# VectorE's softmax tail of one tile moved ahead of the next tile's head

## What is computed

```python
scores = scale * np.matmul(q_c, k_c.transpose(0, 1, 2, 4, 3))
scores = scores - np.max(scores, axis=-1, keepdims=True)
attn = np.exp(scores)
attn = attn / (np.sum(attn, axis=-1, keepdims=True) + 1e-09)
out = np.matmul(attn, v_c)
...
x = out.transpose(0, 2, 1, 3).reshape(B * S, H * D)      # 2304 tokens x 512
# experts: P from x @ w_gate, exp, 8 Sinkhorn steps; out += P[:, e] * (relu(x @ w1[e]) @ w2[e])
# last block: elu(x @ w_in) @ w_out, d_ff = 2048
```

## Time and profile before

| | |
|---|---|
| time, median of 3 runs | 1995.28 us (1994.5 to 1996.69) |
| time of the profiled execution | 1994.76 us |
| its span | 1993.0 us |
| busy in the span: PE, DVE, ACT, POOL | 98%, 56%, 36%, 27% |
| first matmul of the first expert step | 82.66 us from the span's start |

### The profile page before, as it was taken

One profiled execution on the slowest core, in us unless ns is written; L12 is line 12 of the kernel. 1 busy time (PEld: TensorE's weight loads), 2 busy tenths in 40 slices (PEclk: granted clock), 3 DMA queues, 4 the chain that ended last, 5 costly groups with the idle time before them and its releaser, 6 DMA issues.

```text
span 1993.0 us, 30945 instructions
## 1 busy us (share of the span) xinstructions
PE 1946.3 (98%) x10450; PEld 1752.8 (88%) x10450; DVE 1118.8 (56%) x1874; ACT 719.7 (36%) x1516; POOL 531.0 (27%) x600
## 2 busy tenths in 40 slices
PE   6799999999999999999999999999999989999999
PEld 5699999998999889998899988999889868998888
DVE  6666654555545555455554555545555576666666
ACT  4632223322232323332223322233323455555554
POOL 4822252222222222222222222222222352222220
PEclk9999999999999999999999999999999999999999
DMA  9310000000000000000000000000000000000002
GB/s 225 84 36 29 22 22 22 21 21 21 21 21 21 21 21 31 27 26 21 21 21 21 21 21 21 21 21 21 21 21 32 11 22 22 21 21 21 21 21 95
DMA packets 34264, 61.37 MB, mean 31 GB/s; under 512 B 3248, under 2 KB 21680, under 8 KB 34224
## 3 DMA queue, kind: packets, MB, share of 16 engines
q1 hardware_dynamic: 34224, 60.84, 10.4%
HBM read 56.12 MB, written 4.72 MB: 31 GB/s over the span
## 4 chain that ended last, share of the span: by engine, by line
PE 93%; DVE 3%; POOL 2%; ACT 1%; issue 1%; POOLq 0%; DVEq 0%
PE bank L480 44%; PE bank L510 8%; PE bank L497 8%; PE bank L498 8%; PE bank L502 8%; PE bank L511 8%; PE bank L512 8%; POOL prob L312 1%; DVE x_sum L972 1%; POOL x_lo L366 1%; ACT x_hi L718 0%; PE bank L583 0%; DVE x_lo L983 0%; DVE acc L1008 0%; DVE acc L1002 0%
## 5 line engine op out<-in xcount | busy, mean ns | idle before, releaser
L480 PE MATMUL bank<-x_hi,w_hi 128*128 128x384 f32 x1680 | 568.0, 338 | 10.9 <-DVE x_lo L983 6.9
L480 PE MATMUL bank<-x_hi,w_lo 128*128 128x384 f32 x1680 | 565.8, 337 | 0.0
L480 PE MATMUL bank<-x_lo,w_hi 128*128 128x384 f32 x1680 | 563.9, 336 | 0.0
L1008 DVE SCALAR_TENSOR_TENSOR acc<-bank,route,acc 128x512 f32<-128x512 f32 x504 | 354.4, 751 | 285.5 <-PE bank L512 285.5
L744 ACT ACTIVATE h_raw<-bank 128x384 f32<-128x384 f32 x360 | 176.6, 491 | 742.7 <-PE bank L480 740.9
L990 DVE TENSOR_TENSOR h_raw<-bank,h_raw 128x384 f32<-128x384 f32 x360 | 200.7, 558 | 421.0 <-PE bank L480 419.4
L480 PEld LDWEIGHTS bank<-x_hi,w_hi 128*128 128x128 f32 x1680 | 316.2, 188 | 21.7 <-issue 8.9
L480 PEld LDWEIGHTS bank<-x_lo,w_hi 128*128 128x128 f32 x1680 | 316.4, 188 | 5.5
L321 POOL TENSOR_TENSOR w_sum<-raw 128x256 f32<-128x256 f32 x40 | 29.6, 739 | 1089.3 <-PE bank L480 1082.1
L480 PEld LDWEIGHTS bank<-x_hi,w_lo 128*128 128x128 f32 x1680 | 315.9, 188 | 0.0
L510 PE MATMUL bank<-w_hi,h_hi 128*128 128x512 f32 x720 | 281.4, 391 | 3.2 <-DVE h_lo L995 2.1
(11 more groups left out here) (90 smaller groups left out, 1791.3 us busy)
## 6 DMA issues: line engine op xcount, KB each, us to landing
raw<-in_w_up SPq DMA_DIRECT2D x40, 512.0 KB, 3.2
raw<-in_w_down SPq DMA_DIRECT2D x40, 512.0 KB, 3.3
qk<-in_q_k SPq DMA_DIRECT2D x36, 256.0 KB, 6.9
v_wide<-in_v SPq DMA_DIRECT2D x36, 128.0 KB, 5.8
out<-acc SPq DMA_DIRECT2D x18, 256.0 KB, 2.0
gate_w<-in_w_gate SPq DMA_DIRECT2D x1, 16.0 KB, 7.8
```

The lines of the kernel that those rows point to most:

```text
L480: mm = nc.tensor.matmul(up_ps[s], w[:, s, kk, :], xs[:, s, kk, :], start=first and s in (M1, M2, M5), stop=kk == 1 and w is w1_lo, skip_gr ...
L1008: nc.vector.scalar_tensor_tensor(acc[:, t, :], y_ps[i], route_flat[:, bass.ds(EXPERTS * t + expert, 1)], acc[:, t, :], ALU.mult, ALU.add). ...
```

## The change

In VectorE's loop of the attention stage the tail of tile i-1 now stands ahead of the head of tile i. The `x_sums` stay at the end of an iteration, and so now follow a head directly. GpSimd gets one more wait, ahead of the memset of `gate_wide`: for the seven low parts of the first weights, which it has itself issued two iterations earlier (`gate_wide` lies in the same memory as the raw weights that these read).

```diff
                 if i == 8:
-
+                    pool.wait_ge(w1_lo_done, 7)
                     nc.gpsimd.memset(gate_wide[:, :, :].bitcast(F32), 0.0).then_inc(gate_zero, 1)
...
             for i in range(TILES + 1):
+                if i >= 1:
+                    softmax_tail(i - 1)
                 if i < TILES:
                     softmax_head(i)
-                if i >= 1:
-                    softmax_tail(i - 1)
                 if 9 <= i < 13:
                     x_sums(0, 0, ((M5, M6, M7, M3)[i - 9],))
```

## The result

The changed kernel takes **1999.09 us** (median of 11 runs, 1997.51 to 2002.44), the kernel before, run beside it on the same chips, 1994.95 us (11 runs). The ratio is 1.0022, with a 95% interval of 1.0013 to 1.0030: 4.1 us slower. The forecast was 2.5 us slower, 1997.3 us.

The account below looks back on a forecast made before the run. The prediction saw a loop of waits, no engine full, pacing the attention stage. A stage end 2.04 us later plus 0.5 us of low PE clock, on 1994.76, gave 1997.3 us; range 1994.0 to 1999.8.

Parts of the forecast that it names:

- The lead of tiles 0 to 8: Early attention tiles: VectorE's tail no longer waits behind the next subtraction; norm of tile 3 starts 1.49 us earlier.
- The collisions: Tiles 10, 11, 12, 15, 16: x_sum arrives 0.17 us behind POOL's x_low and waits; 4.74 us per tile, before 3.77.
- The clock: End of attention stage: PE's longer pause drops its clock from 78.5 to 81.9, costing 0.5 us (bounds 0 and 3.4).
- the first rival: PE starts the expert steps at the low clock, costing 2.2 us in place of 0.5: 1999.0 us; chance 0.22.
- the x_sum first: Rival in the five colliding tiles: x_sum starts before x_low, saving 0.5 us each: 1994.3 us, no change; chance 0.13.
- Nothing collides: Rival: x_sums slip in without waiting, all tiles about 3.17 us, loads would allow it: 1989.0 us; chance 0.04.

Follow-up runs that it names:

- e4: The changed kernel plus ten identity transposes per iteration ahead of those of prob on PE, iterations 10 to 19; 1997.58 us, ratio 1.0013.
- e8: The changed kernel plus a POOL wait ahead of five x_lows (iterations 10, 11, 12, 15, 16) until that iteration's x_sum is done; 1994.53 us, ratio 0.9998.
- e9: e1 with the last two x_sums (M7, M3 of the second block) moved behind the norm of tile 17; 1992.75 us, ratio 0.9987.
- e1: The kernel before with the tail ahead of the head in iterations 1 to 8 only, old order in 9 to 18; 1994.38 us, ratio 0.9993.

## Why the prediction was right, and where a size was off

- **The lead of tiles 0 to 8**: norm of tile 3 expected at 23.71, measured 23.79; norm of tile 6 37.52 and 37.62; norm of tile 7 41.03 and 41.08. The reciprocal of tile 8 was expected at 42.12 and came at 42.85, since the den lost not only to the norm but also to the memset of `gate_wide` behind it (the first fence above: 1.20 us). That 0.7 us became 0.5 us at the reciprocal of tile 9 (45.65 and 46.12).
- **The collisions**: five x_sums of 2.50 to 2.52 us, 4.75 us per tile (4.74 expected); 3.16 us in tiles 13 and 14 (63.52 to 66.68, expected 3.16); 3.19 in tile 17 (3.18). The last x_sum was 2.56 us late, not 2.04, and the whole 0.5 us is tile 8's den.
- **The clock**: this is the term whose size was off. The step "a low stretch of 3.41 us from 78.5, of which 1.0 us is on the path, costs 0.5 us" was mis-sized. The clock did fall, at 76.76, but stayed low for 13.65 us in the profiled execution, and in the median it cost about 1.8 us (changed kernel against e4). I had carried over the length of the one low stretch seen before, in which PE was busy for 3.10 of 3.41 us. At the end of the stage PE had only short jobs, and the clock did not come back with the first of them. That it would fall at all was in part luck. The forecast had a pause of 3.04 us and the fall 4.37 us behind its start; in the trace the pause was 2.32 us (75.32 to 77.64), hardly longer than the harmless 2.07 of before, and the fall came 1.4 us behind its start. The same trace has a low clock at 63.10, behind no pause above 1.46 us since 52.34. So the length of one pause was the wrong thing to go by. This was the mechanism of the first rival, priced there at 2.2 us.
- **The rivals**: the x_sum first was excluded by the traces of the change itself, and e8 shows what it would have been: 4.31 or 4.32 us per tile (4.24 worked out) and 1994.53 us (1994.3 worked out). Nothing collides was excluded by the same rows. The loads did not come to bound the stage: PE waited for q and k three times in each of the two traces (6.2 us in all before, 6.5 after), and e9, whose stage is the shortest, starts the experts at 80.87.
- **The rule** of the Trainium skill (SBUF — State Buffer, "Who interferes with whom"), that whichever of the two issues first has the shared pair for its whole instruction and blocks the other. The traces agree for an instruction that comes while the other engine's is running: in the changed kernel the x_low was first and the x_sum waited for its end (2.50 to 2.52 us, five times); in e8 the x_sum was first by the added wait, and the den, which came while the x_low ran, waited for that one's end (1.30 or 1.31 us, five times). For one that is already waiting when the other engine's next one comes they do not in every case: see the first point of the last section.

In sum, about 2.3 us of the 4.1 are VectorE's chain (expected 2.0), and about 1.8 us PE's clock (expected 0.5). The measured 1999.09 us lies in the range, but on the first rival's 1999.0 and not on the forecast's 1997.3.

## What to carry to other kernels

Moving a short chain earlier on an in-order engine also moves what stands behind it: here a 0.91 us addition, put from behind a reciprocal to behind a subtraction, arrived 0.11 or 0.12 us after a POOL instruction instead of 0.17 us before one, five times, and these 4.9 us are more than the lead of 3.47 us. So where VectorE and POOL both work on SBUF, write down for every tile which of them starts first, and by how much; a wait that fixes the order (e8), or moving the addition to where nobody waits (e9), was worth more here than the shorter chain of the early tiles (e1). And a longer stage costs more than its length if PE's pauses in it grow, since the work behind it may then begin at half the clock.

## What the hardware showed that was not expected

- A waiting den of 128x8 was not served at the end of the norm that it waited for: the memset behind that norm (42.06 to 42.79) went first, and the den ended at 42.82, 1.20 us after its start in place of 0.17. Behind the attention of the kernel before, a waiting x_sum (96.05, 2.49 us long) seems to have got in between two x_lows: the three of them from 95.16 on took 6.86 us, where three took 5.38 from 78.70 on. Which of the two engines is served at such a boundary stayed open.
- The granted clock stayed at 0.50 for 13.65 us, with PE busy for 11.19 us of them, and the eleven runs spread over 4.9 us in place of 3.1 us before. The three longest (2001.99 to 2002.44 us) have a mean granted clock of 0.990 or 0.991 over the span, the other eight 0.992 to 0.996.
